# Scattering the last expert's sums on their own, splitting the one-hot lanes between VectorE and ScalarE, and loading one function set

## The chip, the cores and the metric

The kernel runs on one core of one Trainium2 chip. The metric is the device time of one execution in microseconds, as the median over several runs. Five engines run side by side: TensorE (PE in the profile, its weight loads PEld), VectorE (DVE), ScalarE (ACT), GpSimd (POOL) and SyncE (SP). They meet only at semaphores. SP, ACT and POOL also issue DMAs, and all of these are carried by the core's 16 DMA engines.

## The reference

Three stages follow each other on 1536 tokens of 512 values:

```python
x = attention(q, k, v)            # window of 16 keys each way plus sums of blocks of 32, head size 64
# first mixture: two experts of eight for each token
noisy = x @ w_gate + log1p(exp(x @ w_noise)) * noise
top2, top2_w = the two largest of noisy, and their softmax
x1[mask] += top2_w * (relu(x[mask] @ w1[e]) @ w2[e])
# second mixture: one expert of eight, and only where the skip score is positive
do_compute = x1 @ w_skip > 0
e_idx = argmax(x1 @ w_gate2);  gate_w = softmax(...)[e_idx]
out = x1;  out[mask] += gate_w * (relu(x1[mask] @ w1b[e]) @ w2b[e])
```

In both mixtures there are 8 experts with weights of 512x1024 and 1024x512. The output is `out`, 1536x512, float32.

## The kernel before

**Stages.** The attention comes first, in 12 tiles of 128 tokens. Its result goes to the DRAM tensor `x_dram` (520 columns: 512 values and 8 gates). Then tokens are routed to experts. Both mixtures gather their tokens from DRAM with indirect DMAs by lists of token numbers and add their outputs back to DRAM with indirect DMAs that accumulate. Products are made of three terms with weights and tokens split in a rounded part (`hi`, made by ACT) and a rest (`lo`, made by DVE).

**Routing.** `route` (DVE, L1584) takes a group of tiles. It finds the experts and the gates, asks PE for the ranks of the tokens within their expert (`ranks`, L768 on), and then makes two one-hot matrices for each tile and pick, in a ring of eight: `lane_hot` (L1700, 128x128, one where the lane equals `lane_f`) and `col_val` (L1702). PE multiplies them (`lists`, L787, matmul L793) and accumulates the lists. `index_lists` (L1706) turns the sums into the index tables `take_ix` and `put_ix`. The first mixture is routed in one group of 12 tiles with two picks (24 pairs of matrices). The second is routed in two groups of six tiles with one pick (6 pairs each). ACT's part is one exponential (`weights`, L1110) and the store of the gates beside the tokens (`store_gates`, L1117). For the first mixture ACT also computes Exp (L1102) and Ln (L1105).

**First mixture.** It runs in rounds of 416 tokens of one expert; with these inputs there are eight rounds, n = 0 to 7. A round has a part with `units` (L839) and `columns` (L845) for hidden units 0 to 3, then the same for 4 to 7. POOL gathers the tokens of a round ahead (`take`, four indirect DMAs at L1350) and adds the results of a round to `x1_dram` one round later (`put`, L1355, four indirect DMAs at L1366: 128, 128, 128 and 32 rows). After the four, POOL waits until they have landed and frees `rows_out` and `ix_put` by the semaphore `yfree`. DVE waits for `yfree` before it copies the next `ix_put` (L1819), late in the round.

**The handover between the mixtures.** The second routing needs the logits of x1, which is complete only after the last expert's put. So SP copies x1 as it is after seven rounds to `part_dram` (L615, four DMAs) as soon as `yfree` says that put 6 is done, then issues the last four weight pieces of that stretch and waits until all but three have landed (`load_piece`, `land`), then waits for the copies and lets POOL make put 7 (`s_may_put`). Then it loads `part_dram` tile by tile into the tile buffers (L626, four buffers; a load waits until PE has turned the tile four before). PE turns each tile (L1038), multiplies it by the router weights (`second_logits`, L759) and turns the result (`turn_logits`, L766). The last expert's share of the logits is computed apart (PE L820, DVE `logits`, L1766), written into columns 512 to 520 of `rows_out`, and so carried to `x1_dram` by put 7 together with the rows. When put 7 has landed POOL raises `s_m1done`. SP then loads these sums as `more_logit` (L631, one DMA for each group of six tiles), and after them copies x1 to `out` (L635, four DMAs of 768 KB). DVE adds both shares in `route` (L1602). PE has its `ranks` for the first group after the step of tile 9 of its loop, so ahead of tile 10. PE's own work goes on behind that in program order.

**Second mixture.** It runs in slots of 128 tokens. POOL's first gather (L1461) waits for the counts, for the stores of the gates (`s_gates`) and for the lists (`s_listed`). PE runs ten `keep_warm` products (L687) and then turns the gathered tokens (L924).

Of the kernel before, what the change touches and what calls it, by code (L numbers as in the profile page):

```python
# [25 lines left out]
F32 = mybir.dt.float32  # L26
# [9 lines left out]
P = 128  # L36
# [15 lines left out]
E = 8  # L52
# [90 lines left out]
def build(nc, q, k, v, m1_gate, m1_noise_w, noise, m1_w1, m1_w2, m2_skip, m2_gate, m2_w1, m2_w2,  # L143
# [14 lines left out]
    with keep:  # L158
# [47 lines left out]
        gates_last = sb("gates_last", [P, PARTS])  # L206
        lane_h = sb("lane_h", [P, P], F16)
# [102 lines left out]
        xg = sb_in(routing, "xg", [P, D + LOGITS])  # L310
# [10 lines left out]
        rows_out = sb_in(rounds, "rows_out", [P, PARTS, D + LOGITS])  # L321
# [41 lines left out]
        s_hot = sem("s_hot")  # L363
        s_list = sem("s_list")
# [18 lines left out]
        s_may_put = sem("s_may_put")  # L383
        s_last_gates = sem("s_last_gates")
# [116 lines left out]

        block = keep.enter_context(nc.Block())
# [13 lines left out]
        def _(eng):  # L516
# [81 lines left out]
            for i in range(N // P):  # L598
                eng.dma_start(x1_dram[i * P:(i + 1) * P, :], zeros).then_inc(s_zero, 16)
            AIR = 4  # L600
            ready = (E + SETS) * PIECES
            base_rows = [slice(i * N // BASES, (i + 1) * N // BASES) for i in range(BASES)]
            for g in range(PIECES, ready):
                if g == ready - PIECES // 2:
# [9 lines left out]
                    for rows in base_rows:  # L614
# [29 lines left out]
        def _(eng):  # L644
# [385 lines left out]
            for t in range(NT + 2):  # L1030
                if t < NT:
# [9 lines left out]
                    last.then_inc(s_x1t, 1)  # L1041
                if 1 <= t <= NT:
# [4 lines left out]
                if t == first[1] + 3:  # L1047
                    ranks(1, first)
# [7 lines left out]
        def _(eng):  # L1056
# [32 lines left out]
            eng.dma_start(noise_sb[:], noise.rearrange("(t p) e -> p t e", p=P)).then_inc(s_router, 16)  # L1089
# [873 lines left out]
```

## Time and profile before

| | us |
|---|---|
| median of 3 runs | 697.62 (693.18, 697.62, 699.52) |
| profiled execution | 695.7, of which the span from first to last instruction is 693.9 |
| PE busy in the span | 633.5 (91%) |
| DVE, ACT, POOL busy | 381.4, 293.2, 206.9 |
| mean granted TensorE clock | 0.965 of 2.4 GHz |

The stages in the span: attention to 110.5 us, first routing to 143, first mixture to 468, handover and second routing to 504, second mixture to 684, last put to 694. The share of busy time is a mean over stages with different limits, so a change is worth what the stage in which it lies says: there one reads which wait ended last. The chain of waits is the list of what released what, followed back from the last instruction.

### The profile page before, as it was taken

The numbers are of one execution on the slowest core, as the hardware profiler recorded it, in microseconds if no ns is written. First come the engines' busy times: TensorE is split into PE (matmuls) and PEld (weight loads), VectorE is DVE, ScalarE is ACT, GpSimd is POOL, SyncE is SP. The second block draws the span as 40 slices with busy tenths as digits, with TensorE's granted clock in tenths as the row PEclk, the third lists the DMA queues.
The fourth block names the chain that finished last, engine by engine and source line by source line (L and its number), as shares of the span: only waits on it lengthen the run. The fifth ranks groups of instructions, "written<-read, shape, count | busy, mean of one in ns | idle before, by whom it ended". The sixth has DMA issues, their size and how long they took to land.

```text
span 693.9 us, 13641 instructions
## 1 busy us (share of the span) xinstructions
PE 633.5 (91%) x4142; PEld 562.3 (81%) x4142; DVE 381.4 (55%) x742; ACT 293.2 (42%) x503; POOL 206.9 (30%) x225
## 2 busy tenths in 40 slices
PE   6688883799999999999999999998699999999993
PEld 6576773489999999999999999986478888788882
DVE  3686787645363545446355544531665677656731
ACT  2365662043253444334243433424164575545620
POOL 1538860220241506033240604203023233131230
PEclk9999997599999999999999999999799999999997
DMA  9999995126182744719272562788546769568130
GB/s 225 205 254 258 265 308 205 47 85 212 51 230 73 179 145 104 237 52 260 64 202 106 135 209 61 221 300 207 164 154 202 224 197 340 165 183 262 32 59 1
DMA packets 98034, 119.39 MB, mean 172 GB/s; under 512 B 57444, under 2 KB 57700, under 8 KB 97968
## 3 DMA queue, kind: packets, MB, share of 16 engines
q1 hardware_dynamic: 80432, 94.04, 44.2%
q0 software_dynamic: 10464, 23.83, 16.0%
q10 hardware_dynamic: 7072, 0.73, 0.7%
q8 instruction: 31, 0.51, 0.3%
q14 instruction: 35, 0.29, 0.1%
HBM read 103.24 MB, written 23.34 MB: 182 GB/s over the span
## 4 chain that ended last, share of the span: by engine, by line
PE 75%; SPq 8%; DVE 5%; DMA 4%; issue 3%; ACT 1%; POOL 1%; POOLq 0%; DVEq 0%; ACTq 0%
PE bank L845 21%; PE bank L839 21%; PE bank L952 19%; SPq L520 5%; SPq L535 2%; PE bank L828 2%; PE bank L808 2%; PE bank L737 1%; PE bank L968 1%; DMA out<-y_sb,ix_put 1%; PE bank L720 1%; PE bank L749 1%; DVE col_val L1702 1%; PE bank L709 1%; DMA xg<-x_moe,ix_take 1%
## 5 line engine op out<-in xcount | busy, mean ns | idle before, releaser
L1544 DVE TENSOR_TENSOR w_lo<-stage,w_hi x120 | 141.6, 1223 | 22.5 <-ACT w_hi L1076 21.9
L1076 ACT CAST w_hi<-stage x120 | 119.6, 1047 | 9.6 <-PE bank L952 9.5
L845 PE MATMUL bank<-unit_hi,w_hi 128*128 128x416 f32 x256 | 92.6, 362 | 0.0
L1795 DVE SCALAR_TENSOR_TENSOR unit_lo<-bank,unit_hi 128x416 fp32r<-128x416 f32 x64 | 37.9, 592 | 97.2 <-ACT unit_hi L1162 97.2
L839 PE MATMUL bank<-tok_hi,w_hi 128*128 128x416 f32 x256 | 90.6, 354 | 0.7 <-DVE bank L1830 0.7
L845 PE MATMUL bank<-unit_lo,w_hi 128*128 128x416 f32 x256 | 90.2, 352 | 0.0
L839 PE MATMUL bank<-tok_hi,w_lo 128*128 128x416 f32 x256 | 89.7, 350 | 0.0
L845 PE MATMUL bank<-unit_hi,w_lo 128*128 128x416 f32 x256 | 89.7, 350 | 0.0
L1162 ACT ACTIVATE unit_hi<-bank 128x416 fp32r<-128x416 f32 x64 | 33.2, 519 | 130.2 <-PE bank L839 130.2
L1366 POOL DMA_INDIRECT x_moe<-rows_out,ix_put x32 | 59.0, 1844 | 57.8 <-DVE rows_out L1783 36.2
L839 PE MATMUL bank<-tok_lo,w_hi 128*128 128x416 f32 x256 | 58.5, 350 | 0.0
L1344 POOL COPY ix_take<-take_ix 128x4 int32 (+1 forms) x8 | 1.5, 185 | 172.7 <-PE bank L808 172.7
L839 PEld LDWEIGHTS bank<-tok_hi,w_hi 128*128 128x128 f32 x256 | 48.0, 188 | 1.7 <-issue 1.1
L845 PEld LDWEIGHTS bank<-unit_hi,w_hi 128*128 128x128 f32 x256 | 48.1, 188 | 1.0
L845 PEld LDWEIGHTS bank<-unit_hi,w_lo 128*128 128x128 f32 x256 | 48.3, 188 | 0.5
L839 PEld LDWEIGHTS bank<-tok_hi,w_lo 128*128 128x128 f32 x256 | 48.1, 188 | 0.4
L845 PEld LDWEIGHTS bank<-unit_lo,w_hi 128*128 128x128 f32 x256 | 48.0, 188 | 0.4
L839 PEld LDWEIGHTS bank<-tok_lo,w_hi 128*128 128x128 f32 x256 | 47.9, 187 | 0.5
L952 PE MATMUL bank<-w_hi,ht_hi 128*128 128x512 f32 x112 | 46.7, 417 | 0.0
L952 PE MATMUL bank<-w_hi,xt_hi 128*128 128x512 f32 x112 | 45.6, 407 | 0.7 <-ACT xt_hi L1204 0.7
L952 PE MATMUL bank<-w_lo,ht_hi 128*128 128x512 f32 x112 | 44.3, 395 | 0.0
L952 PE MATMUL bank<-w_lo,xt_hi 128*128 128x512 f32 x112 | 44.2, 395 | 0.0
(170 smaller groups left out, 1086.4 us busy)
## 6 DMA issues: line engine op xcount, KB each, us to landing
stage<-in_moe_w SPq DMA_DIRECT2D x128, 512.0 KB, 5.7
v_win<-in_v SPq DMA_DIRECT2D x24, 192.0 KB, 5.9
x_moe<-rows_out SPq DMA_DIRECT2D x12, 260.5 KB, 4.6
x_att<-x_sb POOLq DMA_DIRECT2D x12, 256.0 KB, 4.6
x_part<-x_moe SPq DMA_DIRECT2D x4, 768.0 KB, 8.9
rows_in<-x_part SPq DMA_DIRECT2D x12, 256.0 KB, 4.0
out<-x_moe SPq DMA_DIRECT2D x4, 768.0 KB, 8.7
late_raw<-in_v SPq DMA_DIRECT2D x6, 384.0 KB, 7.0
```

The lines of the kernel that those rows point to most:

```text
L520: eng.dma_start(by_token(kind, b)[:, tile], src[:, tile * P:(tile + 1) * P, :].rearrange("h p d -> p h d"))\
L535: eng.dma_start(v_win[NSUM:KEYS, w % WR, :, 0:HD], v[b, :, start:start + WK, :].rearrange("h s d -> s h d"))\
L808: last = eng.transpose(ps[:, i * rows:(i + 1) * rows], rows_in[0:rows, t, i * P:(i + 1) * P], ident[0:rows, 0:rows])
L828: last = eng.transpose(ps_turn[0:PART[t], t * P:(t + 1) * P], out_t[:, PSTART[t]:PSTART[t] + PART[t]], ident)
L839: last = eng.matmul(ps_unit[f % 2][:, 0:W], w, x, start=(i == 0), stop=(i == len(mine) - 1))
L845: last = eng.matmul(ps_out[chunk][:, 0:W], w[:, WC // 2 + f, chunk * P:(chunk + 1) * P], h[:, f % UNITS, :], start=(f == 0 and i == 0), st ...
L952: last = eng.matmul(ps[:], *every[i], start=(i == 0), stop=(i == len(every) - 1))
L1076: eng.copy(piece(w_hi[n % SETS], j), stage[:, j, :]).then_inc(s_hi, 1)
L1162: eng.activation(unit_hi[:, f % UNITS, :], ps_unit[f % 2][:, 0:W], ACT.Relu)\
L1366: eng.indirect_dma_start(x1_dram, bass.IndirectOffsetOnAxis(ap=ix_put[0:rows, t:t + 1], axis=0), rows_out[0:rows, t, :], None, bounds_chec ...
L1544: eng.tensor_tensor(piece(w_lo[n % SETS], j), stage[:, j, :], piece(w_hi[n % SETS], j).bitcast(F32), ALU.subtract)\
L1795: eng.scalar_tensor_tensor(unit_lo[:, f % UNITS, :], ps_unit[f % 2][:, 0:W], 0.0, unit_hi[:, f % UNITS, :].bitcast(F32), ALU.max, ALU.subt ...
```

## The change

1. The logit columns of x1 go to a DRAM tensor of their own, `more_dram` (1536x9). `x1_dram` and `rows_out` shrink from 521 to 520 columns. DVE's `logits` writes into a tile `more_out` and raises `s_sums`; in every round, before the rows, POOL's `put` scatters `more_out` with four more indirect DMAs (zeros in all rounds but the last).
2. SP loads the sums of the first group ahead of tile 11, as soon as the four small scatters have landed, and those of the second group behind it. It no longer waits for `s_m1done` for these. The copies of x1 to `out` still wait for it.
3. ACT's stores of the gates of the second mixture both come after `s_m1done` and after ACT's loop over the tiles. PE's `ranks` of the first group move one tile back, behind the turning of tile 10.
4. Of the one-hot lanes, every second one of the first mixture (12 of 24) and three of the last six of the second are computed by ACT (`lanes`: Square, then Relu, on 128x128), and DVE leaves these out. PE waits for both engines on those.
5. ACT is given one function set at the start, `natural_log_exp_and_others`.
6. One more DMA of zeros fills `more_dram` in the attention.

```diff
-    x1_dram = nc.dram_tensor("x_moe1", (N, D + LOGITS), F32, kind="Internal").ap()
+    x1_dram = nc.dram_tensor("x_moe1", (N, ROW), F32, kind="Internal").ap()
+    more_dram = nc.dram_tensor("x_more", (N, LOGITS), F32, kind="Internal").ap()
...
+        by_act = [2 * t + 1 for t in range(NT)] + [2 * NT + t for t in range(GROUPS[1][1][0], NT, 2)]
...
             for t in range(NT):
+                if t == NT - 1:
+                    all_rounds = eng.snap(total, min_val=1, max_val=E * ROUNDS)
+                    for part in range(PARTS):
+                        eng.wait_ge(s_put_sums[part], all_rounds * 16)
+                    load_sums(0)
                 if t >= XR:
                     eng.wait_ge(s_x1t, t - XR + 1)
                 eng.dma_start(x1_sb[:, t % XR, :], part_dram[t * P:(t + 1) * P, :])\
                    .then_inc(s_x1[t % XR], 16)
+            load_sums(1)
+            land(0)
             eng.wait_ge(s_m1done, 1)
-            for i, (t0, t1) in enumerate(GROUPS[1]):
-                more = x1_dram[t0 * P:t1 * P, D:D + LOGITS]
-                eng.dma_start(more_logit[:, t0:t1, :],
-                              more.rearrange("(t p) e -> p t e", p=P)).then_inc(s_more[i], 16)
-            land(0)
...
                     eng.wait_ge(s_hot, at + 1)
+                    if at in by_act:
+                        eng.wait_ge(s_near, by_act.index(at) + 1)
...
+                if t == first[1] + 4:
+                    ranks(1, first)
                 if 1 <= t <= NT:
                     eng.wait_ge(s_x1te, t)
                     second_logits(t - 1)
                 if t >= 2:
                     turn_logits(t - 2)
-                if t == first[1] + 3:
-                    ranks(1, first)
...
+            eng.preload_act_table_set("natural_log_exp_and_others")
...
+            def lanes(m, group):
+                eng.wait_ge(s_lane, group_no[m, group] + 1)
...
+                def nearness(at):
+                    eng.wait_ge(s_far, by_act.index(at) + 1)
+                    eng.activation(lane_hot[at % HR][:], lane_hot[at % HR][:], ACT.Relu, scale=-1.0,
+                                   bias=1.0).then_inc(s_near, 1)
+                for i, at in enumerate(mine):
+                    t, pick = divmod(at - 2 * m * NT, picks)
+                    if at >= HR:
+                        eng.wait_ge(s_list, at - HR + 1)
+                    eng.activation(lane_hot[at % HR][:], lane_h[:], ACT.Square, scale=-1.0,
+                                   bias=lane_f[:, pick, t:t + 1]).then_inc(s_far, 1)
+                    if i:
+                        nearness(mine[i - 1])
+                nearness(mine[-1])
...
-                if t == first[1] + 4:
-                    store_gates(1, first)
+            eng.wait_ge(s_m1done, 1)
+            store_gates(1, first)
             weights(1, second)
             store_gates(1, second)
+            lanes(1, second)
...
+                    eng.wait_ge(s_sums, n + 2)
+                    eng.wait_ge(S["ix"], n + 1)
+                    eng.sem_inc(S["start"], 1)
+                    for t in range(PARTS):
+                        rows = PART[t]
+                        eng.indirect_dma_start(more_dram,
+                                               bass.IndirectOffsetOnAxis(ap=ix_put[0:rows, t:t + 1],
+                                                                         axis=0),
+                                               more_out[0:rows, t, :], None, bounds_check=N - 1,
+                                               oob_is_err=False, compute_op=ALU.add)\
+                           .then_inc(s_put_sums[t], 16)
                     eng.wait_ge(S["ye"], n * DK + (DK + 2))
...
-                        eng.tensor_scalar(lane_hot[at % HR][:], lane_h[:], lane_f[:, i, t:t + 1],
-                                          None, ALU.is_equal)
+                        if at not in by_act:
+                            eng.tensor_scalar(lane_hot[at % HR][:], lane_h[:], lane_f[:, i, t:t + 1],
+                                              None, ALU.is_equal)
...
-                        last = eng.tensor_scalar(rows_out[0:rows, t, D:D + LOGITS],
+                        last = eng.tensor_scalar(more_out[0:rows, t, :],
                                                  ps_more[0:rows, t * LOGITS:(t + 1) * LOGITS],
                                                  gates_last[0:rows, t:t + 1], None, ALU.mult)
-                    return last
+                    last.then_inc(s_sums, 1)
...
                                 if e == E - 1:
                                     logits(n, dn)
+                                else:
+                                    eng.sem_inc(s_sums, 1)
```

## Rows read from the trace of the kernel before

**Rows 1.** Chain of waits, first routing: start us, us, what

```profile
110.76 1.28 ACT L1105
...
130.73 0.16 DVE lane_hot L1700
130.90 0.23 DVE col_val L1702
```

**Rows 2.** Timeline, handover: PE's loop over the tiles and the second routing

```profile
467.61 1.04 PE L1038 MATMUL bank<-c_late,rows_in 128*128 128x128 f32 x8
...
479.98 0.22 PE L766 MATMUL bank<-c_late,gt_sb 9*128 9x9 f32 x1
...
482.22 2.50 SPq L635 DMA_DIRECT2D out<-x_moe  x4
...
483.23 0.21 DVE L1602 TENSOR_TENSOR logit<-bank,more_logit 128x54 f32<-128x54 f32 x1 [14.57 <-DMA more_logit<-x_moe]
...
485.34 0.20 PE L777 MATMUL bank<-mask_b,before_b 128*128 128x48 bf16 x1 [1.71 <-DVE mask_b L1648]
```

**Rows 3.** Chain of waits, end of the second routing: start us, us, what

```profile
490.30 0.24 PE bank L766
...
499.09 4.60 PE bank L687 x10
```

**Rows 4.** Timeline, SP's queue, 380 to 470 us: start, us in issue, what

```profile
446.11 2.62 SPq L615 DMA_DIRECT2D x_part<-x_moe  x4
...
462.91 6.13 SPq L626 DMA_DIRECT2D rows_in<-x_part  x6
```

**Rows 5.** Timeline, POOL: first and last scatter of put 6, last of put 7

```profile
430.10 1.63 POOL L1366 DMA_INDIRECT x_moe<-rows_out,ix_put  x1 [3.24 <-issue]
...
437.11 1.75 POOL L1366 DMA_INDIRECT x_moe<-rows_out,ix_put  x1 [0.30 <-issue]
...
475.21 1.33 POOL L1366 DMA_INDIRECT x_moe<-rows_out,ix_put  x1 [0.30 <-issue]
```

**Rows 6.** DMA issues at 437, 475, 448, 462, 487 and 499 us: KB each, us to landing

```profile
x_moe<-rows_out,ix_put POOLq DMA_INDIRECT x1, 6.9
...
x_moe<-rows_out,ix_put POOLq DMA_INDIRECT x1, 5.2
...
stage<-in_moe_w SPq DMA_DIRECT2D x1, 512.0 KB, 13.5
...
rows_in<-x_part SPq DMA_DIRECT2D x1, 256.0 KB, 3.9
...
x_moe<-gates ACTq DMA_DIRECT2D x1, 24.0 KB, 8.7
...
xg<-x_moe,take_ix POOLq DMA_INDIRECT x1, 3.4
```

**Rows 7.** Timeline, ACT in the attention: start us, us, engine, line, operation

```profile
64.38 1.26 ACT L1062 ACTIVATE p_sb<-s_sb,nmax 128x120 f32<-128x120 f32 x4
```

**Rows 8.** Lines 1366, 1350 and 1819: duration ns min/median/max, first and last start

```profile
L1366 POOL DMA_INDIRECT x_moe<-rows_out,ix_put x32: 1334/1758/2550, 190.5 to 475.2; - x32
L1350 POOL DMA_INDIRECT rows_in<-x_att,ix_take x32: 929/1019/1116, 142.8 to 425.9; - x32
...
L1819 DVE COPY ix_put<-put_ix x8: 158/160/161, 173.7 to 453.4; 128x4 int32 x8
```

**Rows 9.** Timeline, POOL in the second mixture: one copy at two times

```profile
543.20 1.19 POOL L1429 COPY ix_take<-take_ix 128x1 int32 x1 [8.13 <-DVE gate_next L1856]
...
555.45 0.18 POOL L1429 COPY ix_take<-take_ix 128x1 int32 x1 [5.46 <-DVE gate_next L1856]
```

**Rows 10.** Timeline, DVE, early in the last round

```profile
427.76 0.60 DVE L1766 TENSOR_SCALAR rows_out<-bank,gates_last 128x9 f32<-128x9 f32 x4
...
428.76 0.33 DVE L1783 TENSOR_SCALAR rows_out<-bank,gates_now 32x128 f32<-32x128 f32 x1
```

**Rows 11.** A stretch: us, engines' busy time, TensorE's granted clock, DMA share, GB/s

```profile
494.00:496.00 2.00, 0.00 (x0) 0.00 (x0) 1.68 (x10) 0.00 (x0) 0.00 (x0) 0.63 0.37 56
```

More of the change, by code:

```diff
@@ L206, in build @@
         gates_last = sb("gates_last", [P, PARTS])
+        more_out = sb("more_out", [P, PARTS, LOGITS])
         lane_h = sb("lane_h", [P, P], F16)
@@ L309, in build @@
         xt_hi, xt_lo = [sb_in(routing, f"xt_{part}", [P, DK, P], F32R) for part in ("hi", "lo")]
-        xg = sb_in(routing, "xg", [P, D + LOGITS])
+        xg = sb_in(routing, "xg", [P, ROW])
         y_sb = sb_in(routing, "y_sb", [P, D])
@@ L320, in build @@
         out_t = sb_in(rounds, "out_t", [P, W])
-        rows_out = sb_in(rounds, "rows_out", [P, PARTS, D + LOGITS])
+        rows_out = sb_in(rounds, "rows_out", [P, PARTS, ROW])
         rounds.close()
@@ L363, in build @@
         s_hot = sem("s_hot")
+        s_lane = sem("s_lane")
+        s_far = sem("s_far")
+        s_near = sem("s_near")
         s_list = sem("s_list")
@@ L383, in build @@
         s_may_put = sem("s_may_put")
+        s_sums = sem("s_sums")
+        s_put_sums = [sem(f"m0_put_sums{t}") for t in range(PARTS)]
         s_last_gates = sem("s_last_gates")
@@ L599, in _ @@
                 eng.dma_start(x1_dram[i * P:(i + 1) * P, :], zeros).then_inc(s_zero, 16)
+            eng.dma_start(more_dram.rearrange("(p t) e -> p (t e)", p=P), zeros[:, 0:NT * LOGITS])\
+               .then_inc(s_zero, 16)
             AIR = 4
@@ L622, in _, with load_sums @@
                         eng.snap(total, min_val=0, max_val=E * ROUNDS) * PARTS + (PARTS + 1))
-            for t in range(NT):
+            def load_sums(i):
+                t0, t1 = GROUPS[1][i]
+                eng.dma_start(more_logit[:, t0:t1, :],
+                              more_dram[t0 * P:t1 * P, :].rearrange("(t p) e -> p t e", p=P))\
+                   .then_inc(s_more[i], 16)
+            for t in range(NT):
+                if t == NT - 1:
[3 more added lines that the diff above has]
+                    load_sums(0)
                 if t >= XR:
@@ L1118, in store_gates @@
                    .then_inc(s_gates, 16)
+            def lanes(m, group):
+                eng.wait_ge(s_lane, group_no[m, group] + 1)
+                t0, t1 = group
+                picks = (2, 1)[m]
+                mine = [at for at in by_act if picks * t0 <= at - 2 * m * NT < picks * t1]
+                def nearness(at):
[11 more added lines that the diff above has]
+                nearness(mine[-1])
             def empty_x1(t):
@@ L1248, in _ @@
             store_gates(0, GROUPS[0][0])
+            lanes(0, GROUPS[0][0])
             first_mixture()
@@ L1371, in put @@
                     for t in range(PARTS):
+                        eng.wait_ge(s_put_sums[t], n * 16 + 16)
                         eng.wait_ge(s_put[t], n * 16 + 16)
@@ L1689, in route @@
                 eng.scalar_tensor_tensor(lane_f[:, mine, tiles], block_f[:, mine, tiles], float(-P),
-                                         near[:, mine, tiles], ALU.mult, ALU.add)
+                                         near[:, mine, tiles], ALU.mult, ALU.add).then_inc(s_lane, 1)
                 then(eng.tensor_tensor(col_f[:, mine, tiles], block_f[:, mine, tiles],
@@ L1724, in first_mixture @@
                     eng.wait_ge(s_xst[i], 16 * (NT // 2))
-                eng.memset(rows_out[:, 0:PARTS - 1, D:D + LOGITS], 0.0)
+                eng.memset(rows_out[:, 0:PARTS - 1, D:ROW], 0.0)
+                eng.memset(more_out[:], 0.0)
                 eng.memset(gates_last[:], 0.0).then_inc(s_last_gates, 1)
```

3 lines of the change are left out of this document (1 added, 2 removed).

## The prediction

> **What bounds the kernel now.** I read the busy times of the page first: PE is busy in 91% of the span, and in the rounds and slots of the mixtures the chain of waits is PE's own products, without a gap. There the change touches only engines beside PE. So I went down the chain of waits to the two stretches where it leaves PE. The first is the routing of the first mixture. The chain holds a load of ACT's function table of 1.28 us, and then 24 pairs of DVE instructions, 0.16 us for `lane_hot` and 0.22 to 0.23 for `col_val` [rows 1]. The second is the handover. PE walks over the tiles from 467.61; POOL's put 7 must land before SP may load the sums, DVE starts the second routing at 483.23 released by that load, and PE stands 1.71 us for DVE's mask [rows 2]. Then PE's last turned logits come at 490.3, the second group is routed, ten products of 4.6 us together run at the lower clock, and the slots begin at 503.7 [rows 3]. Last I read what stands just off the path there: SP's copies and loads [rows 4], POOL's puts [rows 5] and the landing times [rows 6]. They decide this case.
>
> **First routing, the table.** Exp, Ln and Exp again now find one set. The first of the two reloads lies on the chain: -1.3 us [rows 1]. The second, behind Ln, is hidden behind DVE's search for the two largest and is worth nothing. The load at the start of the kernel stays. [...]
>
> **First routing, the lanes.** DVE leaves out 12 of 24 `lane_hot`: 12 x 0.16 = 1.9 us [rows 1]. What must keep up is ACT, with two instructions for each of the twelve. I have no Square or Relu of 128x128; the nearest row is the exponential of 128x120, four in 1.26 us, so about 0.3 apiece [rows 7]. That is 0.6 us for a pair against DVE's 0.16 + 2 x 0.225 = 0.61, and ACT may start more than a microsecond earlier, as soon as `lane_f` is made. So ACT about keeps pace: -1.9 us. If its two handshakes made a pair 0.75, the twelve would end 12 x 0.14 = 1.7 us less 1.1 of head start later, and the gain would be 1.3. PE's extra wait lies beside. First routing: -3.2 us, bounds -2.6 and -3.3. All behind it (gather, first round) shifts with it.
>
> **Extra scatters in the rounds.** Each put now begins with four scatters of 36-byte rows. A scatter with addition costs POOL 1.33 to 2.55 us, a gather 0.93 to 1.12, and 0.30 lies between two [rows 5, 8]. How that divides into rows and bytes no row shows. The gather is the lower bound: 4 x 1.32 = 5.3 us. The upper one is put 6 as it ran, 437.11 + 1.75 + 0.30 - 430.10 = 9.1 us [rows 5]. The slowest run while DVE splits weights. A POOL copy in the second mixture, too, takes 1.19 us at one time and 0.18 at another [rows 9]. I take 8.0, near the scatters that run at that place. [...] In rounds 1 to 6 this is paid by nobody: in the last round, laid out like them, put 6 has landed at 437.11 + 6.9 = 444.0 [rows 5, 6] and DVE copies the next `ix_put` at 453.4 [rows 8], 9.4 us later. If that cover were gone DVE, then PE, would wait in seven rounds.
>
> **Put 6 and the copy of x1.** In the last round the same put releases the copy to `part_dram`. The sums are ready at 427.76 + 0.60 = 428.36, the rows at 429.09 [rows 10], so the small scatters start 0.73 earlier than put 6 did, at 429.4. With 8.0 the rows start at 437.4, the fourth three medians and gaps later (3 x 2.06 = 6.2 [rows 8]), at 443.6, and it lands 5.2 to 6.9 later [rows 6], say 6: at 449.6. The copies were issued at 446.11 [rows 4]: 3.7 us late. Behind them the first weight piece needs 13.5 us to land [rows 6], for which SP waits, so this is full DMA time and shifts whole. The tile loads began at 462.91 [rows 4], some 0.4 behind that landing, so they begin 3.3 late, at 466.2. The first tile lands 3.9 later [rows 6], at 470.1, where PE began at 467.6 [rows 2]: PE's loop is 2.5 us late. Bounds: with 5.3 for the scatters put 6 lands at about 446 and nothing is late; with 9.1, rows at put 6's own pace (7.0) and 6.9 for landing, it lands at 452.4, and PE is 5.2 late.
>
> **The loop and the second routing.** Small scatters of put 7 start near 468.9 and have landed by about 480. SP comes to them behind the load of tile 10, so the sums arrive at about 482.5, and DVE also needs PE's turn of tile 5, 480.2 before [rows 2] and 482.7 now. DVE starts near 482.8, its mask is there 2.1 us later, at 484.9, and PE asks for it only at about 486.7, behind tile 10: the stall of 1.71 us is gone [rows 2]. Tile 11's load, now queued behind the wait, is issued at about 483 and is needed at 488; it is covered. So PE leaves the loop 2.5 - 1.7 = 0.8 us late. Three lanes less on DVE give 3 x 0.16 = 0.5 back. The lists would end +0.3.
>
> **The gates.** The rows of put 7 now follow four scatters. POOL is undisturbed there (rows issued every 1.87 us), so +7.5 less the earlier start 0.73: the landing moves from 475.21 + 5.2 = 480.4 to 487.2 [rows 5, 6], and with it `s_m1done` and the 3 MB from x1 to `out`, issued from 482.22 before [rows 2], from 489.0 now (4.6 later instead of 6.8 if a small scatter costs as a gather). ACT waits there too; its loop ends at about 491, so only the stores of the gates are queued behind it, and `weights` of the second group is not reached. But the first store, issued at 487.2, needed 8.7 us, against 3.4 for the first gather: it landed 13.7 us after the copies began, when they drained [rows 2, 6]. The same 13.7 behind 489.0 is 502.7, behind 486.8 it is 500.5. POOL's first gather asks for all the gates; before, it was only the lists, at 498.8. I take 502.0: the gather starts 0.84 later and lands 3.4 after that [rows 6], at 506.2. PE turned it at 503.7. Handover: +2.6 us, not +0.3, since the later of the two decides.
>
> **Sum.** -3.2 + 2.6 = -0.6 us. The profiled execution took 695.7, 1.9 under the median of 697.62 and inside the three runs; -0.6 makes it 695.1, and the median 697.0. The shorter rows (520 columns), the DMA of zeros (SP's queue, in the attention, hidden by 30 us) and the semaphore counts are at nothing.
>
> **Rivals.**
> - *The handover pays nothing.* Small scatters cost POOL as gathers do and land quickly, the copies to `out` hold no gates back. For it: the sums are 1/58 of the bytes. Against: a scatter of a quarter of the rows still costs 1.33 us [rows 8], so bytes and rows are not the whole price; and the 8.7 us [rows 6]. Then the stall and the lanes are gained whole: -3.2 - 1.7 - 0.5 = -5.4, median 692.2. Chance 0.25.
> - *The clock falls before PE's loop (slower).* PE is idle from the end of the first mixture until tile 0 lands. Once it had run out at the end of its loop, at 490.5, the granted clock fell to 1.2 GHz at about 494.5 [rows 3, 11], 4 us later. If put 6 lands so late that PE stands idle as long before its loop, the loop starts at that clock. The ten products of 4.6 us ran at it [rows 3]; as much work at half speed costs 2.3 us. With PE 5.2 late: -3.2 + 5.2 - 1.7 - 0.5 + 2.3 = +2.1, median 699.7. It decides from about 451 for the landing of put 6. Chance 0.15.
> - *The set isn't used.* The exponential or Ln reloads all the same: +1.3 on the forecast, 698.3; the trace of before can't exclude it. Chance 0.1.
> - The forecast, within 1.5 us of -0.6: 0.5.
>
> **Range and chances.** The bounds of the unknown costs reach from 692.2 to 699.7; the three runs alone lie 6 us apart, so I add a little: 691.5 to 701.0. The forecast's own range is 695.5 to 698.5. About 1% (7 us) is what a measurement of this kernel can tell from no change. No case reaches it, and only their piling up with the spread of the runs could: faster 0.09, same 0.84, slower 0.07.
>
> **What the profile of the changed kernel would show.** One table load on ACT instead of three. The lists of the first mixture in about 7.4 us instead of 9.4. In the timeline of POOL eight scatters for a put; the four small ones in 5.3 (rival one) to 9 us. The copies to `part_dram` issued near 450 and the first turn of the loop near 470, both less the 3.2 us of the first routing (all times above are in the clock of before). No wait of PE for the mask, and instead POOL's first gather of the second mixture waiting for the stores of the gates rather than for the lists. I would be wrong if small scatters cost far less than the gathers, if the copies to `out` let the gates pass, or if DVE's wait for `yfree` showed in the rounds.

## The result

| | before | after |
|---|---|---|
| median of 9 runs, us | 696.37 (693.18 to 699.52) | 701.31 (697.87 to 707.45) |
| profiled execution: time, span | 695.7, 693.9 | 697.9, 695.9 |
| mean granted clock | 0.965 | 0.955 |
| PE, ACT, POOL busy | 633.5, 293.2, 206.9 | 638.2, 298.7, 253.8 |

Ratio of the times 1.0063, 95% interval 1.0039 to 1.0086: 4.9 us slower in the medians, 0.3 us outside the predicted range on its upper side, and in the other direction than forecast. (The prediction started from 697.62, the median of the first three runs of before; 696.37 is that of nine.) The profiled execution of after is the fastest of its nine, so its profile understates the loss.

The rest is told with five marks of the profile: the end of the attention (ACT's exponential of the first routing), the first product of round 0, the tile loads of the last stretch, the turn of the first gathered tile of the second mixture ("first turn"), and the first product of that slot's second layer ("slot").

| profiled, us | attention ends | to round 0 | round 0 to first turn | round 0 to slot | slot to end | span |
|---|---|---|---|---|---|---|
| before | 110.5 | 32.5 | 360.5 | 368.4 | 182.5 | 693.9 |
| after | 114.6 | 29.6 | 362.5 | 371.4 | 180.4 | 695.9 |
| difference | +4.1 | -2.9 | +2.0 | +2.9 | -2.1 | +2.0 |

I had said -3.2 for the second column and +2.6 for the handover (third column). The fourth holds the third and the clock behind it. The first column, in which I had looked at nothing, holds the loss; one profile alone can't show it, since attentions of equal kernels end up to 6 us apart (table below), and the experiments must.

**The attention.** SP's key loads come first. Before: DMA issues of the first 60 us (KB each, median us to landing), then stretches of the timeline (us, busy time of PE, PE's weight loads, DVE, ACT, POOL with instruction counts, granted clock, DMA share, GB/s).

```profile
stage<-in_k SPq DMA_DIRECT2D x6, 256.0 KB, 4.8
```
```profile
8.00:16.00 8.00, 6.50 (x47) 5.70 (x45) 4.87 (x8) 3.23 (x6) 1.11 (x4) 1.00 1.14 250
16.00:24.00 8.00, 6.50 (x103) 5.56 (x100) 6.49 (x10) 2.50 (x8) 6.63 (x11) 1.00 1.17 207
```

The same of after:

```profile
stage<-in_k SPq DMA_DIRECT2D x6, 256.0 KB, 6.8
```
```profile
8.00:16.00 8.00, 4.58 (x32) 3.88 (x30) 2.87 (x5) 3.07 (x6) 0.00 (x0) 1.00 1.38 198
16.00:24.00 8.00, 7.03 (x60) 6.40 (x61) 6.43 (x11) 0.18 (x2) 6.61 (x11) 0.57 1.16 246
```

The loads land 2.0 us later, PE does 32 products instead of 47 between 8 and 16 us, and the granted clock then falls to 0.57, where it was 1.00. (The profile gives the clock as a share of full speed, and all clocks here are such shares; the 1.2 GHz of the prediction and of one expectation stand for the share of 0.50, as the profile of before shows it from 496 to 504 us.) It falls in before too, only later (0.79 from 24 to 32 us); over the first 106 us it is 0.92 in after and 0.97 in before. No line of the change touches these loads.

**The first routing.** The trace of after shows that Exp and Ln find one set. Before loads a table three times: at 6.24 us, ahead of Ln [rows 1] and ahead of the second Exp (start us, us, engine, line, operation):

```profile
6.24 1.28 ACT L490 ACT_TABLE_LOAD   x1 [6.24 <-issue]
...
112.05 0.28 ACT L1105 ACTIVATE z_sp<-z_exp 128x96 f32<-128x96 f32 x1
112.35 1.28 ACT L1110 ACT_TABLE_LOAD   x1
```

After loads one in the whole span, at the line that names the set (L1115), and none stands around Ln (L1131) or ahead of the second Exp (L1136):

```profile
6.64 1.28 ACT L1115 ACT_TABLE_LOAD   x1 [6.64 <-issue]
...
114.59 0.25 ACT L1128 ACTIVATE z_exp<-bank 128x96 f32<-128x96 f32 x1 [1.15 <-PE bank L771]
114.87 0.28 ACT L1131 ACTIVATE z_sp<-z_exp 128x96 f32<-128x96 f32 x1
118.74 0.28 ACT L1136 ACTIVATE top_e<-top_d 128x96 f32<-128x96 f32 x1 [3.58 <-DVE top_d L1677]
```

DVE's walk over the lists leaves out every second `lane_hot`. Chain of waits of after (start us, us, what), the answer to [rows 1]:

```profile
124.57 0.25 DVE lane_hot L1764
124.82 0.45 DVE col_val L1766 x2
125.27 0.16 DVE lane_hot L1764
125.43 0.45 DVE col_val L1766 x2
...
131.52 0.23 DVE col_val L1766
131.80 0.51 PE bank L817 x2
```

From 124.57 to 131.75 are 7.2 us; I had said 7.4.

**The handover.** SP and POOL, timelines of after (start, us in issue or busy), the answer to [rows 4, 5]:

```profile
448.93 2.65 SPq L627 DMA_DIRECT2D x_part<-x_moe  x4
...
464.90 15.99 SPq L651 DMA_DIRECT2D rows_in<-x_part  x11
481.16 0.37 SPq L638 DMA_DIRECT2D more_logit<-x_more  x1
...
488.83 2.58 SPq L657 DMA_DIRECT2D out<-x_moe  x4
```
```profile
430.39 1.63 POOL L1416 DMA_INDIRECT x_more<-more_out,ix_put  x1 [2.31 <-DVE more_out L1831]
...
437.93 2.18 POOL L1428 DMA_INDIRECT x_moe<-rows_out,ix_put  x1 [0.30 <-issue]
...
444.55 1.34 POOL L1428 DMA_INDIRECT x_moe<-rows_out,ix_put  x1 [0.30 <-issue]
```

The chain of waits of after, from PE's loop to the second mixture, the answer to [rows 2, 3]:

```profile
464.90 4.31 DMA rows_in<-x_part
...
469.34 1.55 PE bank L1062 x8
470.89 1.81 PE bank L781 x8
...
481.16 4.87 DMA more_logit<-x_more
...
488.24 0.20 PE bank L799
...
492.70 0.24 PE bank L788
...
496.17 5.95 DMA x_moe<-gates
...
503.13 3.48 DMA xg<-x_moe,take_ix
...
506.66 0.67 PE bank L948 x4
...
507.99 2.08 PE bank L976 x4
```

A transfer stands on the chain that was not there before: the second store of the gates, 5.95 us, and behind it the first gather. Off the chain, PE's timeline shows the mask's stall, 1.71 us before [rows 2], and the new wait for the gather:

```profile
488.24 0.20 PE L799 MATMUL bank<-mask_b,before_b 128*128 128x48 bf16 x1 [0.85 <-DVE mask_b L1711]
...
506.66 0.65 PE L948 MATMUL bank<-c_late,xg 128*128 128x128 f32 x4 [1.57 <-DMA xg<-x_moe,take_ix]
```

### The profile page after: what moved, and what is told of

It reads as the page before. It is cut to its first block, busy times and chain, and to the rows that moved or that the text cites. A ratio compares the mean times of both kernels' runs of the same rounds, so it can differ in the third digit from the quotient of the medians.

```text
span 695.9 us, 13779 instructions
## 1 busy us (share of the span) xinstructions
PE 638.2 (92%) x4142; PEld 567.2 (81%) x4142; DVE 379.0 (54%) x728; ACT 298.7 (43%) x531; POOL 253.8 (36%) x257
## 4 chain that ended last, share of the span: by engine, by line
PE 76%; SPq 9%; DMA 6%; DVE 3%; issue 3%; POOL 1%; ACT 0%; POOLq 0%; DVEq 0%; ACTq 0%
PE bank L976 23%; PE bank L863 19%; PE bank L869 18%; SPq L530 6%; SPq L545 2%; PE bank L832 2%; PE bank L852 2%; DMA stage<-in_moe_w 2%; PE bank L992 2%; PE bank L759 1%; PE bank L781 1%; PE bank L709 1%; PE bank L742 1%; PE bank L771 1%; PE bank L948 1%
## 5 line engine op out<-in xcount | busy, mean ns | idle before, releaser
L1607 DVE TENSOR_TENSOR w_lo<-stage,w_hi x120 | 141.7, 1222 | 22.2 <-ACT w_hi L1100 18.8
L1416 POOL DMA_INDIRECT x_more<-more_out,ix_put x32 | 51.5, 1610 | 42.2 <-DVE more_out L1831 26.3
L1428 POOL DMA_INDIRECT x_moe<-rows_out,ix_put x32 | 55.2, 1726 | 9.8 <-issue 9.8
```

The lines of the kernel that those rows point to most:

```text
L1416: eng.indirect_dma_start(more_dram, bass.IndirectOffsetOnAxis(ap=ix_put[0:rows, t:t + 1], axis=0), more_out[0:rows, t, :], None, bounds_ch ...
L1428: eng.indirect_dma_start(x1_dram, bass.IndirectOffsetOnAxis(ap=ix_put[0:rows, t:t + 1], axis=0), rows_out[0:rows, t, :], None, bounds_chec ...
L1607: eng.tensor_tensor(piece(w_lo[n % SETS], j), stage[:, j, :], piece(w_hi[n % SETS], j).bitcast(F32), ALU.subtract)\
```

## The experiments

All ratios are to the kernel before, which ran beside each group of experiments with medians of 696.5, 696.9 and 696.8 us.

| kernel | attention ends | to round 0 | round 0 to first turn | round 0 to slot | slot to end | median us | ratio (95%) |
|---|---|---|---|---|---|---|---|
| before + 36 floats | 118.2 | 32.3 | 360.7 | 368.4 | 181.5 | 702.5 | 1.0096 (1.0064 to 1.0128) |
| before + 64 floats | 109.2 | 32.7 | 360.6 | 368.5 | 182.7 | 697.5 | 1.0013 (0.9986 to 1.0040) |
| padded | 107.8 | 29.0 | 362.1 | 371.9 | 181.1 | 695.5 | 0.9987 (0.9960 to 1.0014) |
| padded, again | 111.1 | 29.2 | 361.9 | 371.7 | 181.8 | 694.1 | 0.9965 (0.9940 to 0.9991) |
| sums alone, padded | 109.2 | 32.0 | 362.2 | 369.7 | 180.7 | 698.0 | 1.0022 (0.9991 to 1.0054) |
| lanes and set alone | 108.5 | 29.6 | 362.3 | 370.2 | 182.9 | 693.6 | 0.9945 (0.9918 to 0.9973) |
| last put alone | 114.0 | 29.0 | 362.3 | 371.9 | 184.0 | 699.8 | 1.0054 (1.0021 to 1.0086) |
| last put alone, again | 109.5 | 28.8 | 363.3 | 372.8 | 184.6 | 698.2 | 1.0019 (0.9994 to 1.0043) |
| last put, late copies | 113.0 | 28.8 | 358.6 | 366.1 | 183.5 | 690.6 | 0.9928 (0.9896 to 0.9960) |
| the same, PE kept busy | 111.3 | 29.0 | 361.2 | 368.7 | 183.1 | 693.6 | 0.9940 (0.9912 to 0.9968) |
| **padded, late copies** | 110.7 | 28.9 | 358.5 | 366.0 | 181.8 | 689.7 | **0.9903** (0.9870 to 0.9935) |
| lanes and set, late copies | 113.5 | 28.9 | 360.1 | 367.9 | 182.4 | 694.6 | 0.9942 (0.9908 to 0.9976) |

**Where the attention's time went: the place of a tile.** The theory: `more_out` stands ahead of `stage` in SBUF. Its 36 floats are 144 bytes, rounded up to 160, of every partition, so `stage` and what follows it move from byte 20224, a multiple of 256, to 20384, which is none. The rival: chance, or the new table set and the lanes. The first experiment adds only a tile that nobody uses to the kernel before.

```diff
+        spare_tile = sb("spare_tile", [P, PARTS, LOGITS])
```


> The kernel before with one edit: an unused tile of 36 floats per partition is allocated where the change allocates more_out. Nothing reads or writes it. It moves all tiles behind it (the stage buffer for q, k and the weights, late_raw, kt, v_win) up by 160 bytes, so that the stage buffer no longer starts on a multiple of 256 bytes (20384 instead of 20224). Theory L (layout): the loads of q and k into the stage, whose runs are 256 bytes, land later (6.8 instead of 4.8 us median), PE idles at the start, its clock falls, and the attention ends about 4 us later, at 114.5 instead of 110.5; the whole kernel is slower by 3 to 5 us, ratio 1.004 to 1.007. Rival N (chance): the 4.1 us lost in the attention of the changed kernel are scatter between executions; then this kernel's attention ends at 110.5 and the ratio is 1.000, within 0.002. [...]

Measured: ratio 1.0096, where 1.004 to 1.007 had been expected, and more than the whole change. Everything behind the attention is as before, and the key loads and the clock are those of after:

```profile
stage<-in_k SPq DMA_DIRECT2D x6, 256.0 KB, 6.8
```
```profile
8.00:16.00 8.00, 4.89 (x32) 4.18 (x30) 2.96 (x5) 3.17 (x6) 0.00 (x0) 1.00 1.38 198
16.00:24.00 8.00, 7.03 (x72) 6.67 (x72) 6.52 (x11) 0.27 (x2) 6.63 (x11) 0.79 1.15 240
```

So it is neither chance nor the table set. The queue's lines for 1 to 8 us tell what changed. Before, then the kernel with 36 floats more (packets, MB, share of the 16 DMA engines):

```profile
q1 hardware_dynamic: 3846, 1.00, 64.1%
```
```profile
q1 hardware_dynamic: 2962, 0.78, 70.3%
```

A share of 16 engines over 7 us is 112 us: 71.8 us for 3846 packets is 18.7 ns for one, 78.7 us for 2962 is 26.6 ns. The packets are the same size (1.00 MB / 3846 = 260 bytes, 0.78 MB / 2962 = 263), and on average they take 1.4 times as long. Not each of them does: by the durations in the traces, 73% of the 256-byte packets in this window still take under 20 ns (before: 99%), and the median is 18 ns in both. One in twenty takes 60 ns or more (before: one in a thousand), and these hold 70% of what is added.

The control moves the same tiles by 256 bytes, so that the multiple is kept.

```diff
+        spare_tile = sb("spare_tile", [P, 64])
```


> The kernel before with one unused SBUF tile of 64 floats in front of `stage` and the tiles behind it: they move by 256 bytes per partition and stay on multiples of 256. Theory (alignment): a shift that keeps the multiple costs nothing: ratio 1.000, within 0.003; attention ends at 107 to 111 us, `stage`<-`in_k` lands in 4.8 us. Rival (any shift, or any tile more, costs, for instance by another order of tiles): as with 36 floats, ratio 1.0096, landing 6.8 us, attention ends near 118. If the ratio is 1.000, the 5 to 6 us of the run with 36 floats are those of the alignment alone.

Measured: ratio 1.0013, landing 4.8 us, attention to 109.2. A larger shift (256 bytes, ratio 1.0013) costs nothing that shows, where one of 160 cost 1.0%, so it is the place that costs and not the shift. The landing is the sure sign of it: 6.8 us in the two profiles with the 36 floats, 4.8 to 5.0 in all twelve without. The clock and the count of products are not; both were as low in some of the twelve. Three things no run here tells: why a few packets took 60 ns and more at such a place and most were as fast as before, whether a multiple of 64 or 128 would do (160 is neither), and which of the tiles behind `more_out` matters, since all of them move.

**The change without the shift.** The changed kernel with `more_out` padded to 64 floats per partition ("padded" in the table):

```diff
-        more_out = sb("more_out", [P, PARTS, LOGITS])
+        more_wide = sb("more_wide", [P, PARTS, 16])
+        more_out = more_wide[:, :, 0:LOGITS]
...
-                eng.memset(more_out[:], 0.0)
+                eng.memset(more_wide[:], 0.0)
```


> The changed kernel with one edit: more_out is a part of a tile of 64 floats per partition instead of 36, so that all tiles behind it move by 256 bytes and the stage buffer starts on a multiple of 256 again. Theory L: the attention ends at 110.5 as in the kernel before and the kernel takes 4 us less than the changed one (which had the ratio 1.0063), so a ratio of 0.999 to 1.001. Rival N: as the changed kernel, ratio 1.006.

Measured: 0.9987, and 0.9965 when it ran again beside other kernels, on which more below. The intervals of the first and of the change itself (1.0039 to 1.0086) don't meet. The padding takes away 0.8 to 1.0%, 5 to 7 us, what the unused tile had cost; what is left of the change lies, by the two ratios, 0.9 to 2.4 us below before, where I had forecast 0.6.

**The two halves.** First the table set and ACT's lanes alone, on the kernel before (the lines of the change that belong to them, of which the main ones stand here), then the scattered sums alone, padded.

```diff
+        by_act = [2 * t + 1 for t in range(NT)] + [2 * NT + t for t in range(GROUPS[1][1][0], NT, 2)]
...
+            eng.preload_act_table_set("natural_log_exp_and_others")
...
+            lanes(0, GROUPS[0][0])
...
+            lanes(1, second)
```


> The kernel before with only parts 4 and 5 of the change: half the lanes on ACT and one function set. No tile is added, the layout is that of before. By the forecast's steps the first routing is 3.2 us shorter (2.9 in the trace of the changed kernel) and the second 0.5: ratio 0.995. If a rival holds by which the first round starts when it did (the gather or the weights not being ready), 1.000.

```diff
-        by_act = [2 * t + 1 for t in range(NT)] + [2 * NT + t for t in range(GROUPS[1][1][0], NT, 2)]
+        by_act = []
...
-            eng.preload_act_table_set("natural_log_exp_and_others")
...
-            lanes(0, GROUPS[0][0])
...
-            lanes(1, second)
```


> The changed kernel without lanes on ACT and without the one function set, in the aligned layout: only the separate scatter of the sums, with its scatters in every round, the later stores of the gates and the later copies to out. If the handover costs what the trace of the changed kernel shows (PE's first slot 3.1 us late, of it 1.4 by the clock at the start of the loop and 1.4 by the clock at the first slot, less 0.5 for the lanes there), this is 2 to 4 us slower than before, ratio 1.003 to 1.006. By the first rival of the prediction, the handover gains 1.7: ratio 0.9975.

Measured: 0.9945, as expected, and 1.0022, less than the 1.003 to 1.006 expected and more than the rival's 0.9975. Together they make 0.9967, beside 0.9987 and 0.9965 for the whole. The first half has the routing (29.6 us against 32.5); the second has nothing to show for its work, 1.5 us in the medians and not clear of zero. In the profile of the sums alone the mask's stall is 1.52 us. It follows the time in which the sums' load lands: 5.5 us there, 4.9 in after (stall 0.85), 4.3 to 4.6 in the padded kernels (0.25 to 0.47), and 5.8 in the last experiment (1.67). The handover of the lanes alone was 1.8 us longer than that of before, with no part of the change in it but the lanes, and I read no more from one profile than that.

**Is it put 6?** I had priced the four extra scatters of put 6 as a delay that shifts whole. In this version of the padded kernel only the last put scatters the sums:

```diff
-                        eng.wait_ge(s_put_sums[part], all_rounds * 16)
+                        eng.wait_ge(s_put_sums[part], 16)
...
-                def put():
+                def put(with_sums=False):
...
+                    if with_sums:
...
-                        put()
+                        put(back == 1)
```


> The changed kernel with its tile padded to 64 floats, and the four small scatters only in the last put of the first mixture, which is the only one that carries the last expert's sums (here the last expert has one round): puts 1 to 6 scatter rows alone. Theory: put 6 is back at its own time, so the copies to `part_dram` start 303.2 us behind round 0 as before (the changed kernel: 304.8) and the tile loads as before (319.95 against 320.7): 0.8 to 1.6 us gained against the padded kernel, ratio to before 0.996 to 0.998. Put 7 with its eight scatters is as it was, so the gates still land late and the first gather of the second mixture still waits for them. Rival (put 6 had slack): the same time as the padded kernel, 0.9987.

Measured: 1.0054, slower than the padded kernel, where it was to be faster. The copies to `part_dram` were issued 303.3 us behind round 0 (before 303.2, padded 304.5), as expected, but the tile loads at 319.9 in this one, in the padded one, and before. So the 1.3 us by which put 6 was late had slack: the rival was right. The excess lies elsewhere, and ran once more beside the padded kernel to see whether it was chance.

> The changed kernel with its tile padded, once more, on one chip with the next: its earlier ratio was 0.9987 (0.996 to 1.0014). Expected 0.997 to 1.001. It is here because the run with the scatters in the last put alone came out at 1.0054 where less work had been expected to give 0.997.

> The run with the scatters in the last put alone, once more (1.0054 before, 1.0021 to 1.0086). Theory (granted clock by chance: its profile lost time in the attention and at the second mixture's first slot, where the clock stood at 1.2 GHz, not at put 6, which was 1.3 us earlier as expected): it returns to within 0.003 of the padded kernel. Rival (leaving the scatters out is slower by its own doing, for instance by putting the first slot where the clock falls): again 1.004 to 1.008, with the low clock at the first slot of the second mixture again.

Measured: 0.9965 and 1.0019, again 4 us apart. So it isn't chance alone; neither the theory (within 0.003 of the padded kernel) nor the rival (1.004 to 1.008) fits the second number. Nearly 3 us of it are in "slot to end". Two of them come early: in the two profiles one slot takes 14.6 and 15.2 us instead of 12.5, because POOL's first put of the second mixture starts later. The others, 1.2 or 1.3 us, lie behind the last slot (last section). The timeline of POOL, this kernel and then the padded one:

```profile
518.62 1.33 POOL L1500 DMA_INDIRECT xg<-x_moe,ix_take  x1 [0.86 <-POOL ix_take L1497]
528.34 1.62 POOL L1513 DMA_INDIRECT out<-y_sb,ix_put  x1 [8.38 <-issue]
```
```profile
519.43 1.33 POOL L1496 DMA_INDIRECT xg<-x_moe,ix_take  x1 [0.86 <-POOL ix_take L1493]
523.91 1.62 POOL L1509 DMA_INDIRECT out<-y_sb,ix_put  x1 [3.15 <-issue]
```

8.38 us against 3.15, with no wait that the profile shows ("issue"); DVE had `y_sb` ready at 522.0. The gather for slot 3 is queued behind that put, and PE waits for it (2.4 us). The pause is in all four profiles of kernels that scatter the sums only in the last put (9.18, 8.38, 7.14, 6.89 us) and is 3.15 us in the ten others, so it belongs to that program and isn't chance. One thing more sets the four apart. In each, a load of instructions of 8 KB starts within the pause, 1.9 or 2.0 us before the put; in none of the ten does one lie between the gather and the put. Here it is from 526 to 528 us (packets, MB, share of the 16 DMA engines):

```profile
q14 instruction: 1, 0.01, 1.0%
```

So POOL probably waits for its own program, which this edit lengthened and branched differently. That is argued from the order of events; no run separates it.

**Are the gates held by the copies to `out`?** SP issues the four copies only when PE has turned the first tile of the second mixture. Nothing else waits for them before the first put of that mixture.

```diff
             eng.wait_ge(s_m1done, 1)
+            eng.wait_ge(slot_sems["xtp"], 2)
             for rows in base_rows:
```


> As the run before (scatters only in the last put), and SP issues the four copies of 768 KB from x1 to `out` only when PE has turned the first tile of the second mixture. Theory (the stores of the gates are held by these copies): the gates' stores land in 2.5 to 4 us instead of 6 to 9, the first gather is released by the lists again, and PE turns the first gathered tile about 358.5 to 360 us behind round 0 (before 360.5, changed 362.5, padded 362.1): 2 to 3 us gained against the run before, ratio to before 0.992 to 0.995. The copies then share the DMA engines with the second gather, and the first put of the second mixture waits for them: if that is too late, PE stalls at the third slot and the gain is gone. Rival (the gates land late for another reason, such as their own 1536 short rows): the stores still take 6 to 9 us, ratio as in the run before.

Measured, on top of the version above: 0.9928, 9 us less in the median than its first run, on the same chip. The first turn comes 358.6 us behind round 0 instead of 362.3, and the slot 366.1 instead of 371.9. Then the same line on the padded kernel, which isolates it, and on the kernel before with lanes and set:

> The changed kernel with its tile padded to 64 floats (scatters in every put, as in the change), and the four copies to `out` only when PE has turned the first tile of the second mixture. Theory (the copies to `out` hold the gates' stores, and these the first gather, which is the whole cost of the scattered sums): 2 to 4 us less than the padded kernel alone, ratio to before 0.993 to 0.996; the stores land in 2.5 to 3.5 us, PE turns the first gathered tile 358.5 to 359.5 us behind round 0 (padded: 362.1). Rival (the gain of the earlier run came from leaving the scatters out of puts 1 to 6): ratio 0.9987, as the padded kernel.

> The kernel before with the function set and the lanes of ACT only (ratio 0.9945 alone), the sums carried by the rows as before, and the copies to `out` behind the first turn of the second mixture. In this kernel the lists, not the gates, release the first gather, so theory: the copies held nobody there; ratio 0.992 to 0.995, the gather lands about 360 behind round 0 as before. If it comes out below 0.991 the copies also cost the kernel before something (the gather's or the clock's time), and the late copies, not the sums, are the improvement. Rival (the sums ahead of the last tile are worth their 1 to 2 us once the gates are free): the run with padded tile and late copies is 1 to 2 us faster than this one.

Measured: 0.9903 against 0.9965 for the padded kernel beside it, 4.4 us; and 0.9942 against 0.9945, nothing, as far as intervals of 0.3% to either side tell. So the copies cost the kernel whose gates are stored late, and no cost of them shows in the other. In the padded kernel a store of the gates stood on the chain, and then the gather:

```profile
489.74 7.80 DMA x_moe<-gates
...
498.55 3.54 DMA xg<-x_moe,take_ix
...
503.93 2.07 PE bank L977 x4
```

With the late copies no transfer stands there (chain of waits, start us, us, what):

```profile
492.65 0.23 DVE col_val L1768
492.93 0.29 PE bank L819
...
493.98 4.15 PE bank L711 x10
498.13 0.60 PE bank L950 x4
```

DVE's lists release PE, PE's ten products end at 498.1, and the gathered tile is there. Both stores of the gates land in 2.0 us, where they took 10.2 and 7.8 in the padded kernel. The sums may be worth something after all: once the gates are free, the kernel with them is at 689.7 us (6 runs) and the one without at 694.6 (9 runs), on one chip. Their intervals overlap (0.9870 to 0.9935 and 0.9908 to 0.9976), so this is likely and not shown. The profiles have 2.0 us of it from round 0 to the slot, where the rival had said 1 to 2; 2.8 us lie in their attentions, where they are the same code.

**The clock at the handover.** The gates cost more than their wait. Stretches of the padded kernel, and then with late copies (columns as above):

```profile
494.00:498.00 4.00, 3.33 (x8) 2.69 (x9) 1.12 (x4) 0.00 (x0) 0.00 (x0) 0.52 0.53 138
498.00:502.00 4.00, 0.67 (x3) 0.19 (x1) 0.00 (x0) 0.00 (x0) 1.10 (x1) 0.90 0.23 67
502.00:506.00 4.00, 3.19 (x9) 2.40 (x10) 1.46 (x4) 2.42 (x3) 0.75 (x2) 0.50 0.00 2
```
```profile
494.00:498.00 4.00, 4.00 (x10) 2.94 (x10) 0.58 (x2) 0.00 (x0) 1.10 (x1) 0.57 0.23 67
498.00:502.00 4.00, 3.33 (x16) 2.58 (x16) 1.99 (x4) 2.59 (x3) 1.27 (x2) 1.00 0.48 156
502.00:506.00 4.00, 4.00 (x21) 3.23 (x21) 1.97 (x3) 2.27 (x4) 0.00 (x0) 1.00 0.98 295
```

In both, the ten products run at a granted clock of 0.50 (494 to 497 us, stretches of 1 us), and it is back at 1.00 from 498. In the padded kernel PE then waits for the gather, with 0.67 us of work from 498 to 502, and the clock falls a second time, to 0.61 from 501 and 0.50 from 502 us, over the first slot. From the first turn to the slot that kernel takes 9.8 us, this one 7.5: 2.3 us beside the 3.4 by which the turn is earlier.

The last experiment tried to keep the clock up ahead of PE's loop, where it fell to 0.57 in after (470 to 474 us; eight `second_logits` products took 1.81 us there and 0.97 later).

```diff
+            keep_busy(12, ps_unit[1])
             first, second = GROUPS[1]
```


> As the run before, and PE turns the identity twelve times (0.8 us) in the gap between the last round of the first mixture and its loop over the tiles, where it stands idle for 1 to 2 us and where the granted clock fell to 0.52 at 470 us in the changed kernel (1.4 us lost) but not in the padded one. Theory (the idle time before the loop lets the clock fall in part of the executions): up to 0.7 us in the mean, ratio to before 0.001 below that of the run before. Rival (the clock falls for a reason other than this gap, or by chance): no difference within 0.0015.

Measured: 0.9940 against 0.9928 without it: no gain, as the rival said. The clock stood at 1.00 ahead of and in the loop of both profiles, so what it could have bought wasn't there, and the twelve products (1.47 us), which come behind the last round's own, made the loop start 1.3 us later. Why the clock fell there in after stays open.

## Why the prediction was wrong

- **The step that failed** is the last sentence of the sum: "The shorter rows (520 columns), the DMA of zeros (...) and the semaphore counts are at nothing." It lists what the change does beside its four parts and leaves out that it declares one tile more in SBUF, ahead of others. That tile alone, unused, is +1.0% (6 us) on before, and padding it takes 5 to 7 us off after; it is the only term that moves the result out of the range. No rival had it, since all of them lay behind the attention. What I called "all behind it shifts with it" held; what lay ahead I took as untouched, because no instruction there was.
- **First routing**: -3.2 forecast, -2.9 in after, -2.9 with this part alone. One table load of 1.28 us instead of three, ACT kept pace (its pairs begin 0.6 us apart), the lists took 7.2 us. Right in each term; the rival in which the set isn't used is out, since after has no load between Exp, Ln and Exp.
- **Small scatters**: 8.0 us for four at put 6, measured 7.5 (430.39 to 437.93), at put 7 7.2 (469.90 to 477.14). Nearest to my value and not to the gather's 5.3. Over the kernel line L1416 has 1610 ns apiece and the rows' line L1428 1726, and at put 7, undisturbed, both have 1.56 and 1.57 us for 128 rows: 36 bytes a row cost POOL what 2080 cost. The slowest scatter of rows in before, 2.55 us at 432.03, ran beside a split (from 431.89). The small ones hardly slowed so: at put 6 the second and the fourth ran into splits (from 432.93 and from 435.18) and took 1.59 and 1.53 us (1.57 and 1.33 at put 7), while the rows' scatters behind them took 2.18 and 1.98.
- **Put 6 and the copy**: 3.7 us late forecast, 1.6 measured (448.93 less the 1.2 us by which round 0 is later), since the scatters were 0.5 shorter and put 6 landed 4.2 us after its last scatter instead of 6. "Shifts whole" was wrong: the loads were 0.8 late in after and not at all in the padded kernel. The slack lies with the weight pieces: in before SP waited for these ahead of the copies, which went out at 446.1 although put 6 had landed at 444.0, and in after it waited 2.9 us for POOL. The loop then began 0.5 late, not 2.5, but ran its first two tiles at the low clock (0.57 from 470 to 474 us), some 1.4 us.
- **The mask's stall**: said to be gone; 0.85 us were left in after, because the sums' load took 4.9 us and not the 2.5 or so that I had for it, and 0.25 and 0.40 in the two profiles of the padded kernel. Mechanism right.
- **The gates**: right. In the clock of before (1.2 us less) the copies to `out` went out at 487.6 (489.0 forecast), the last store landed at 500.9 (502.0), the first gather waited for it, and the first tile was turned at 505.5 (506.2): +2.0 against +2.6. (The working gives 2.5 from the 503.7 it started from, and 2.7 from the 503.5 of the timeline; it changes nothing.) I had not priced the clock that falls behind that wait, another 0.9 us in after and 1.9 in the padded kernel (third column to fourth). This is the term to which the second rival (a low clock behind an idle PE) pointed, but ahead of the slot. Ahead of the loop the clock did fall in after (0.57), without the rival's condition: the copies went out at 447.7 in the clock of before, not behind 451, and PE waited 0.54 us for the first tile, behind a last round that ended as in before, with one gap of 0.68 us. In the two profiles of the padded kernel it didn't fall there.
- **The first rival**, that the handover pays nothing (-5.4 us), is what the late copies make of it: the handover is 2.4 us shorter than before there, where the rival had 2.2, and the median 7.1 us below before. It needed one more line.
- Without the shift my sum of -0.6 us would have met 0.9 to 2.4 us below before, both within 1%. In part that would be luck. In the padded profiles the routing gave 3.3 to 3.5 us, the handover up to the slot cost 3.3 to 3.5 and not 2.6, and "slot to end", which I had left out, gave back 0.8 to 1.4.

## What to carry to other kernels

A new tile in SBUF moved the tiles declared behind it (`stage` from byte 20224 to 20384). Where transfers write short runs (260 bytes here) into one of them, try to keep its start where it was to a multiple of 256 bytes, by padding the new tile, which took 0.8 to 1.0% off here, or declaring it last (not tried, nor was a smaller multiple); a control with an unused tile of the same size tells in one run what a shift costs. When a change delays a small store, look at which large transfers other engines issue at that moment: four copies went out at 484.0 us that nobody needed before a put at 523.9, and issuing them 15 us later gave 4.4 us back, and the best version here, padded and with late copies, takes 689.7 us, 1.0% less than before.

## What was not expected of the hardware

- Packets of about 260 bytes took 26.6 instead of 18.7 ns of a DMA engine on average when the tiles that they are written to start 160 bytes off a multiple of 256. Most were as fast as ever (73% under 20 ns against 99%); a few long ones, 5% at 60 ns and more, made the difference.
- A wait of 3.5 us behind the ten products (they end at 498.7 in the padded kernel, and the turn begins at 502.1) was followed by a second fall of the clock (1.00 from 498 to 501 us, 0.50 from 502), and from the turn to the slot it took 2.3 us more.
- From the last put to the end it takes 8.2 to 8.3 us in the five profiles of kernels that scatter sums in every put with their copies early or late, and 10.3 to 10.7 in the nine others. The put starts 0.9 to 1.0 us later behind DVE in the five, so about 1.1 us are left: from the last slot to the end 17.7 us against 18.8 to 19.1. What shortens the tail is not known.
- The attention of the kernels whose tiles keep the multiple ended between 107.8 and 114.0 us in the profiles, with dips of the clock at different places. A difference of one profile's attention says nothing below 6 us, and it took the medians of repeated runs to tell the shift.
